# A chain of attention, routed experts and a dense layer on one core: the transfers of v issued by ScalarE instead of SyncE

## What is computed

```
scores = scale * (q_c @ k_c^T)          # per chunk of 64 positions, scale 1/8
attn   = exp(scores - max) / (sum + 1e-9)
x      = attn @ v_c                     # laid out as (2304, 512)
P      = exp(x @ w_gate - max), 8 rounds of dividing by row sums and column sums
y      = sum over e of P[:, e] * (relu(x @ w1[e]) @ w2[e])
h      = y @ w_in
out    = where(h > 0, h, exp(h) - 1) @ w_out
```

## Time and profile before

| | us |
|---|---|
| median of 3 runs | 2099.07 |
| lowest, highest | 2098.47, 2101.9 |
| the profiled execution | 2098.22 |
| its span, first to last instruction | 2096.4 |
| PE busy in the span | 1979.5 (94%) |
| DVE, ACT, POOL busy | 1104.1, 721.5, 557.7 |

### The profile page before, as it was taken

How to read it: one execution, slowest core, us unless ns; L and a number is a source line. 1 busy time by engine, 2 the same in 40 slices (tenths; PEclk the granted TensorE clock), 3 DMA queues, 4 the chain that set the end, 5 groups by cost and what they waited for, 6 DMA issues and landing times.

```text
span 2096.4 us, 30917 instructions
## 1 busy us (share of the span) xinstructions
PE 1979.5 (94%) x10450; PEld 1779.1 (85%) x10450; DVE 1104.1 (53%) x1860; ACT 721.5 (34%) x1516; POOL 557.7 (27%) x610
## 2 busy tenths in 40 slices
PE   4447999999999999999999999999999989999999
PEld 3336898998999989989989899899899978988988
DVE  3224566555455555555554555555555576666666
ACT  2224222233322322333223223323232355554554
POOL 1336223423222222222222222232222283222221
PEclk8668999999999999999999999999999999999999
DMA  4220100000100000001000000000000000000002
GB/s 121 76 76 21 41 21 21 21 20 20 40 20 20 20 20 20 20 20 34 26 20 20 20 20 20 20 30 30 20 20 20 21 21 21 20 20 20 20 20 90
DMA packets 36856, 61.37 MB, mean 29 GB/s; under 512 B 3536, under 2 KB 21968, under 8 KB 36816
## 3 DMA queue, kind: packets, MB, share of 16 engines
q1 hardware_dynamic: 36816, 60.85, 8.8%
HBM read 56.12 MB, written 4.72 MB: 29 GB/s over the span
## 4 chain that ended last, share of the span: by engine, by line
PE 88%; issue 5%; DVE 2%; POOL 2%; ACT 1%; SPq 1%; DMA 0%; POOLq 0%; ACTq 0%
PE bank L447 41%; PE bank L465 8%; PE bank L466 8%; PE bank L470 8%; PE bank L479 8%; PE bank L480 8%; PE bank L478 8%; DVE x_sum L934 1%; POOL prob L281 1%; POOL x_lo L335 1%; POOL w_lo L312 0%; DMA k_wide<-in_k 0%; PE bank L553 0%; DVE h_raw L985 0%; DVE acc L958 0%
## 5 line engine op out<-in xcount | busy, mean ns | idle before, releaser
L447 PE MATMUL bank<-x_hi,w_hi 128*128 128x384 f32 x1680 | 567.2, 338 | 12.9 <-ACT h_raw L714 9.7
L447 PE MATMUL bank<-x_hi,w_lo 128*128 128x384 f32 x1680 | 565.9, 337 | 0.0
L447 PE MATMUL bank<-x_lo,w_hi 128*128 128x384 f32 x1680 | 564.4, 336 | 0.0
L958 DVE SCALAR_TENSOR_TENSOR acc<-bank,route,acc 128x512 f32<-128x512 f32 x504 | 350.2, 747 | 149.7 <-PE bank L480 149.7
L714 ACT ACTIVATE h_raw<-bank 128x384 f32<-128x384 f32 x360 | 176.8, 491 | 670.4 <-PE bank L447 656.6
L940 DVE TENSOR_TENSOR h_raw<-bank,h_raw 128x384 f32<-128x384 f32 x360 | 200.7, 557 | 288.9 <-PE bank L447 286.6
L447 PEld LDWEIGHTS bank<-x_hi,w_hi 128*128 128x128 f32 x1680 | 316.7, 189 | 24.6 <-issue 7.8
L447 PEld LDWEIGHTS bank<-x_lo,w_hi 128*128 128x128 f32 x1680 | 316.7, 188 | 9.7
L290 POOL TENSOR_TENSOR w_sum<-raw 128x256 f32<-128x256 f32 x40 | 29.6, 741 | 1103.7 <-PE bank L447 1096.9
L447 PEld LDWEIGHTS bank<-x_hi,w_lo 128*128 128x128 f32 x1680 | 316.4, 188 | 0.0
L478 PE MATMUL bank<-w_hi,h_hi 128*128 128x512 f32 x720 | 282.3, 392 | 4.4 <-DVE h_lo L990 4.4
(11 more groups left out here) (89 smaller groups left out, 1858.1 us busy)
## 6 DMA issues: line engine op xcount, KB each, us to landing
raw<-in_w_up SPq DMA_DIRECT2D x40, 512.0 KB, 3.2
raw<-in_w_down SPq DMA_DIRECT2D x40, 512.0 KB, 3.2
q_t<-in_q SPq DMA_DIRECT2D x18, 256.0 KB, 3.2
k_wide<-in_k SPq DMA_DIRECT2D x36, 128.0 KB, 3.2
v_wide<-in_v SPq DMA_DIRECT2D x36, 128.0 KB, 2.8
out<-acc SPq DMA_DIRECT2D x18, 256.0 KB, 2.0
gate_w<-in_w_gate SPq DMA_DIRECT2D x1, 16.0 KB, 4.0
```

Source lines behind the costliest of these rows:

```text
L447: mm = nc.tensor.matmul(up_ps[s], w[:, s, kk, :], xs[:, s, kk, :], start=first and s in (M1, M2, M5), stop=kk == 1 and w is w1_lo, skip_gr ...
L958: nc.vector.scalar_tensor_tensor(acc[:, t, :], y_ps[i], route_flat[:, bass.ds(EXPERTS * t + expert, 1)], acc[:, t, :], ALU.mult, ALU.add). ...
```

## The change

The two transfers of v and the wait before them go from SyncE's load_tile to a new function load_v of ScalarE. ScalarE waits once for the operands of tile 0 (qk_loaded[0]) and then issues the v of tiles 0 to 2; in its loop it issues the v of tile i, for 3 <= i < 18, behind x_copy(i-3). The wait on values_done goes with it. The buffers, the semaphores, the addresses and sizes of the transfers and all computations are the same.

```diff
--- before.py
+++ after.py
@@ -240,11 +240,6 @@
                 for g in range(2):
                     half = slice(HD * g, HD * g + HD)
                     sp.dma_start(k_wide[j][half, :, g, :, :], k[t, half, :, :, :]).then_inc(qk_loaded[j], 16)
-                if i >= 3:
-                    sp.wait_ge(values_done, i - 2)
-                for g in range(2):
-                    half = slice(CHUNK * g, CHUNK * g + CHUNK)
-                    sp.dma_start(v_wide[j][half, :, g, :, :], v[t, half, :, :, :]).then_inc(v_loaded[j], 16)
 
             for i in range(TILES):
                 load_tile(i)
@@ -790,6 +785,17 @@
                 nc.scalar.activation(gate_rows[b % 2][:, :], gate_ps[b % 2][0:2 * EXPERTS, 0:BLK], ACT.Copy)\
                     .then_inc(gate_rows_done, 1)
 
+            def load_v(i):
+                t, j = VISIT[i], i % 3
+                if i >= 3:
+                    act.wait_ge(values_done, i - 2)
+                for g in range(2):
+                    half = slice(CHUNK * g, CHUNK * g + CHUNK)
+                    act.dma_start(v_wide[j][half, :, g, :, :], v[t, half, :, :, :]).then_inc(v_loaded[j], 16)
+
+            act.wait_ge(qk_loaded[0], 48)
+            for i in range(3):
+                load_v(i)
             for i in range(TILES + 3):
                 if i < TILES:
                     exp_of(i)
@@ -797,6 +803,8 @@
                     e_copy(i - 2)
                 if i >= 3:
                     x_copy(i - 3)
+                if 3 <= i < TILES:
+                    load_v(i)
                 if i == 4:
                     w1_highs(0)
                 if i == 6:
```

## The result

| | before | changed |
|---|---|---|
| median | 2099.94 us | 2009.14 us |
| lowest, highest | 2098.47, 2101.9 | 2007.95, 2018.78 |
| profiled execution (span) | 2098.22 (2096.4) | 2018.78 (2017.0) |
| first product of the experts starts at | 174.80 | 84.89 |

The ratio is 0.9576, with a 95% interval of 0.955 to 0.9602. The medians are 90.8 us apart; I had forecast 2011, a gain of 88. The execution that was profiled is itself 9.4 to 10.8 us longer than the other three.

A forecast was written before the change was run, and what follows sets the result against it. Bound: q and k queued on SyncE behind v's wait for the values. 15.7 + 4.4 + 17.5 + 5 + 31.2 put tile 17's scores at 73.8 us, 87.7 us earlier: total 2011 us, range 2001 to 2034.

The forecast's parts named there:

- What bounded the kernel: Attention loop: SyncE's wait for v holds the next q and k; 5.8 us of issue and landing in 10.2 a tile.
- The start: Loads before the scores of tile 3: 3.95 MB take 13.6 us, so tile 3 starts at about 15.7 us, not 18.60.
- The price of an issue: Each v issue moved to ScalarE costs 0.6 us, as on SyncE: 1.2 us a tile.
- (c): ScalarE's attention round: 1.6 us of work, 2.8 with two issues, 3.55 with a piece of x_high.
- The period of tiles 3 to 8: Attention rounds without x_high: 3.5 us each after a first of 4.4, plus 5 us extra from the first weights' split.
- The period of tiles 9 to 17: Later attention rounds: several engines' loops at 3.4 to 3.55 us wait on each other, taken as 3.9 us each.
- my candidates: Possible next bounds of an attention round: PE 2.65 us, softmax loop 3.5, ScalarE 3.55, POOL 3.4 (with DMA 2.9).
- The sum: Start and attention rounds added: scores of tile 17 start at 73.8 us in place of 161.51, 87.7 us earlier.
- The clock: PE's granted clock during attention: 1.00 for most of the stretch, near it from some 25 us on.
- Rival 3: Loads in attention: only issue time is saved, 1.2 us on 15 tiles, 18 us; total 2081; chance 0.03.
- Rival 2: ScalarE in attention: an issue costs 2 us, making it the bound at 5.6 and 6.3 us; total 2042; chance 0.12.
- 4: ScalarE in attention: an issue holds the engine until its transfer lands, 13.5 us a round; slower, 2148; chance 0.02.

The follow-up runs named there:

- e1: Changed kernel, ScalarE issuing v, but with SyncE's wait for the values of tile i-3 kept behind k of tile i: 2100.43 us.
- e8: Kernel before the change, all issued by SyncE, v of tile i-2 with its wait behind q and k of tile i: 2007.44 us.
- e4: Changed kernel with the gate's and first group's weights issued behind q and k of tile 4 instead of tile 2: 2004.44 us.
- e5: Changed kernel with v in four transfers of 32 partitions instead of two of 64, so four issues a tile on ScalarE: 2010.44 us.
- e3: Changed kernel with three buffers for soft instead of two: 2009.61 us.
- e6: Kernel before the change, with 22 unread 128x128 products ahead of each scores wait from tile 3 on, keeping PE busy: 2079.3 us.
- e10: Changed kernel, weights behind tile 4, first weights' split spread, pauses between POOL's scalings, v of tile i-2 issued by SyncE: 2004.41 us.
- e2: Kernel before the change, all issued by SyncE, v of tile i-1 with its wait behind q and k of tile i: 2036.37 us.
- e9: Changed kernel with the seven x_low pieces of pair 0 moved from steps 10 to 16 to behind the last prob: 2014.35 us.

## Why the prediction was right, step by step

**What bounded the kernel**: right, and shown by e1. With the wait kept, nothing is gained; e8 shows it from the other side.

**The start: wrong.** I had tile 3 at 15.7, from the bytes up to its own k. It started at 19.39. SyncE, freed of its wait, had by then also issued q and k of tiles 4 and 5 (1.05 MB), and the engines work on all that is issued: 5.0 MB at 290 GB/s end 17.2 us after 2 us. The window 15 to 20 us shows them full, at 260 GB/s. A median landing of 4.2 us for k, in place of the 3.2 I used, says the same. e4, with 1.07 MB of weights moved behind, has tile 3 at 14.97.

**The price of an issue**: 0.6 us on ScalarE's queue (median 0.63), right. That it all adds to the engine's round, (c), was too much: the part beside x_copy is free, 0.66 us a round is not, and ScalarE's round was 3.77 us less 0.59 of waiting, 3.2 in place of 3.55. It had slack for two issues more (e5).

**The period of tiles 3 to 8**: 3.5 and 5 us of disturbance, 26.9 us from tile 3 to tile 9 with the round at the lower clock. Measured 24.65: an undisturbed round was 2.6 to 3.4 us, the first 4.35, and the disturbances stood where I had put them, 5.6 us from tile 6 to 7 and 5.8 from 8 to 9, 4.2 behind.

**The period of tiles 9 to 17**: 3.9 assumed, 3.63 measured. It was set by none of my candidates as written. POOL was listed at 3.4 as free of other waits; with the hand-over that VectorE can only make once x_lo is over, it is 3.77 where x_sum lies beside prob, and 3.18 where it does not. Two rounds at 3.55 and 3.65 in between became shorter with a third buffer of soft (e3).

**The sum**: tile 17 at 73.11, forecast 73.8; an error of +3.7 at the start and of -4.4 behind it cancelled. From there to the first product 11.8 us, in place of 13.3. The total was right to 2 us, its terms were not. The mechanism held; that the number came so near is luck.

**The clock**: 1.00 in nearly all of the stretch, as expected, 0.83 in one window (40 to 50 us), behind the round in which PE stood idle for 3.1 us. e6 prices the low clock at 21 us in the loop as it was before; what the same low clock would cost in the shorter rounds no run shows.

**Rival 3** (only issue time saved) was priced at 2081. As e1 it exists and is worth nothing: 2100. **Rival 2** and **4** rest on a price that was not there.

**Behind 84.89** the profiled execution took 1932.1 us against 1921.6, in line with the long h_lo below. The other three were not traced, but their totals leave no room for it: 2008.96 is 90 us under 2099, the whole gain of the attention.

## What to carry to other kernels

Read for each transfer what stands ahead of it in its queue, not what it itself waits for: q and k waited for a condition written for v, and the cost was the full latency in each round. To free them it did not matter who issues v, only how many rounds the wait lies ahead of the use; one round was not enough (2036), two were (2007), as long as the rounds lasted 3.8 us (with those of e10 q and k were late again). An issue holds what stands behind it in its queue for 0.6 us, but not what the engine has already been handed (e5). Take stock of the bytes in flight before adding transfers to a busy start, and count as part of an engine's round the hand-overs that another engine can only make when it is done.

## What the runs showed of the hardware

POOL held VectorE back for the length of a whole series of its instructions. In the profiled execution of the changed kernel (the last eleven of twelve scalings of acc that POOL ran in a row, VectorE's h_lo of 128x384, then PE's product that waited for it):

```profile
299.22 11.07 POOL L338 TENSOR_TENSOR acc<-acc,route 128x512 f32<-128x512 f32 x11
299.56 11.13 DVE L953 SCALAR_TENSOR_TENSOR h_lo<-h_raw,h_hi 128x384 fp32r<-128x384 f32 x1 [1.42 <-ACT h_hi L718]
```

```profile
310.75 1.65 PE L465 MATMUL bank<-w_hi,h_lo 128*128 128x512 f32 x3 [7.66 <-DVE h_lo L953]
```

h_lo takes 0.56 us in the median; here it takes 11.13 and ends with POOL's series (299.22 + 11.07 = 310.29, 310.69), and PE waits 7.66 us. The profile of e1, whose execution was also some 10 us long, has the like: 11.11 us. In the other nine profiles of kernels without pauses, e2 to e9 and the one before, the longest h_lo of this form is 1.39 to 1.41 us, and their executions are not long; in e3 the h_lo beside the same series takes 1.15 us and gets in behind one scaling. The same happens on a small scale in the rounds of the attention with an x_lo beside it, where L922 ends with x_lo. The Trainium skill, "SBUF — State Buffer", section SBUF: two separate sides, says that VectorE with two inputs in SBUF and GpSimd share a port pair as an exclusive lock, held for the full instruction. The rows on h_lo, which reads h_raw and h_hi, agree with a lock. One instruction is not all it can cost: here the loser was not let in for eleven of POOL's in a row, of which the section does not speak. L922 has one input, so the case of two inputs does not cover it, and by what it is held no trace shows. Why h_lo is let in between two of them in most executions and not in these two stays open.
